# The last 256 tokens' output: copied and stored in two halves, the first while TensorE works on the second

## The reference

```python
# B, H, S, D = 4, 8, 576, 64; tokens = B*S = 2304; d_model = 512; d_ff = 2048
x = attention_with_memory(q, k, v, M_prev, z_prev, beta)    # (2304, 512)
h = x @ w_in1;  g = where(h >= 1, h, where(h <= -1, 0, (h + 1)**2 / 4));  x = g @ w_out1
h = x @ w_in2;  g = maximum(0.01 * h, h);                                 out = g @ w_out2
```

## Time and profile before

| | |
|---|---|
| median of 3 runs | 1002.1 us (1001.63 to 1003.18) |
| the profiled execution | 1002.58 us |
| its span, first to last instruction | 1000.8 us |
| PE busy | 992.4 us (99% of the span) |
| DVE, ACT, POOL busy | 446.2, 512.6, 425.4 us |
| last product ends, copies start, stores are issued | 995.72, 995.75, 996.47 us |

### The profile page before, as it was taken

The page is one execution under the profiler, slowest core; times in us unless marked ns, Lnnn a source line. Parts: engine busy times, 40 slices in busy tenths (PEclk is TensorE's granted clock), DMA queues, the critical chain, the costliest instruction groups (busy, mean ns, idle before and its releaser), DMA issues.

```text
span 1000.8 us, 16729 instructions
## 1 busy us (share of the span) xinstructions
PE 992.4 (99%) x6236; PEld 872.1 (87%) x6236; DVE 446.2 (45%) x1117; ACT 512.6 (51%) x1120; POOL 425.4 (43%) x375
## 2 busy tenths in 40 slices
PE   9999999999999999999999999999999999999997
PEld 6889999989999999999999998888888888888897
DVE  6788756666657656666422274112111111211111
ACT  6787776867677676767534374222222222322121
POOL 3478656564554546455422286222222222222221
PEclk9999999999999999999999999999999999999999
DMA  7762322332313324132110453002000200200010
GB/s 223 221 185 78 92 61 64 81 79 70 91 50 83 81 59 103 50 83 61 39 45 22 119 197 105 22 1 60 5 22 0 64 22 1 64 1 1 1 43 22
DMA packets 98290, 66.77 MB, mean 67 GB/s; under 512 B 74272, under 2 KB 87840, under 8 KB 98208
## 3 DMA queue, kind: packets, MB, share of 16 engines
q1 hardware_dynamic: 96896, 61.23, 22.4%
q10 hardware_dynamic: 1312, 4.46, 1.3%
HBM read 54.53 MB, written 11.07 MB: 66 GB/s over the span
## 4 chain that ended last, share of the span: by engine, by line
PE 90%; ACT 2%; POOL 2%; issue 2%; DVE 2%; DMA 1%; ACTq 0%; DVEq 0%; POOLq 0%
PE Hp L715 13%; PE Hp L716 13%; PE Hp L717 13%; PE Yp L739 7%; PE Yp L740 7%; PE Yp L745 7%; PE At L739 6%; PE At L740 6%; PE At L745 6%; PE At L636 4%; PE At L664 4%; PE At L555 3%; PE At L606 1%; ACT prob L773 1%; POOL Gl L1387 1%
## 5 line engine op out<-in xcount | busy, mean ns | idle before, releaser
L1387 POOL TENSOR_TENSOR Gl<-Gl_raw,Gh 128x512 fp32r<-128x512 f32 x144 | 192.3, 1336 | 435.9 <-ACT Gh L980 435.7
L715 PE MATMUL Hp<-Xh,WAh 128*128 128x256 f32 (+1 forms) x704 | 214.6, 305 | 0.0
L716 PE MATMUL Hp<-Xl,WAh 128*128 128x256 f32 (+1 forms) x704 | 212.7, 302 | 0.0
L717 PE MATMUL Hp<-Xh,WAl 128*128 128x256 f32 (+1 forms) x704 | 212.6, 302 | 0.0
L1221 DVE TENSOR_TENSOR Gl_raw<-Hp,Gl_raw 128x512 f32<-128x512 f32 x72 | 49.8, 692 | 297.5 <-ACT Gl_raw L972 297.5
L972 ACT ACTIVATE Gl_raw<-Hp 128x512 f32<-128x512 f32 x72 | 43.1, 598 | 230.4 <-PE Hp L717 230.4
L715 PEld LDWEIGHTS Hp<-Xh,WAh 128*128 128x128 f32 x704 | 134.0, 190 | 8.3 <-issue 0.4
L716 PEld LDWEIGHTS Hp<-Xl,WAh 128*128 128x128 f32 x704 | 134.1, 191 | 7.7
L980 ACT ACTIVATE Gh<-Gl_raw 128x512 fp32r<-128x512 f32 x144 | 90.9, 631 | 94.1 <-DVE Gl_raw L1221 52.3
L717 PEld LDWEIGHTS Hp<-Xh,WAl 128*128 128x128 f32 x704 | 134.0, 190 | 5.0
L739 PE MATMUL Yp<-WBh,Gh 128*128 128x512 f32 x320 | 132.5, 414 | 0.0
(11 more groups left out here) (159 smaller groups left out, 1936.3 us busy)
## 6 DMA issues: line engine op xcount, KB each, us to landing
raw<-long SPq DMA_DIRECT2D x16, 480.0 KB, 4.0
WAl_raw<-w_in SPq DMA_DIRECT2D x12, 512.0 KB, 4.9
WBl_raw<-w_out SPq DMA_DIRECT2D x12, 512.0 KB, 3.8
Vs_raw<-v_long SPq DMA_DIRECT2D x16, 320.0 KB, 3.6
yT_scratch<-xraw SPq DMA_DIRECT2D x36, 128.0 KB, 2.5
prob<-yT_scratch SPq DMA_DIRECT2D x9, 512.0 KB, 4.2
out<-prob SPq DMA_DIRECT2D x34, 128.0 KB, 2.2
bc<-rn_scratch SPq DMA_DIRECT2D x32, 128.0 KB, 3.3
```

Of the source, the lines that this page charges most:

```text
L715: pe.matmul(h, WAh[:, f, j, :], xh, start=(j == 0), stop=False)
L716: pe.matmul(h, WAh[:, f, j, :], xl, start=False, stop=False)
L717: last = pe.matmul(h, WAl[:, f, j, :], xh, start=False, stop=(j == DT - 1))
L1387: gp.tensor_tensor(Gl[:, U % 2, :], act[:, U % 2, :], Gh[:, U % 2, :].bitcast(F32), ALU.subtract).then_inc(g_lo, 1)
```

## The change

For the last unit of all (`ends`), `output` takes the products in another order: first the two pairs from `Gh` of t = 0 (tick 0), then, after the wait for `g_lo`, the two products from `Gl` of t = 0, the last of which raises the new semaphore `first_done`; then the two pairs and the two low products of t = 1. DVE waits for `first_done` and copies `Yp[:, 0, :]` (semaphore `first_out`); ACT copies `Yp[:, 1, :]` at the end (`y_out`). `store_last(eng, t, e)` now is one store: the 64 partitions 64e to 64e + 63 of one half `y2[:, t, :]`, to a view of `out` with the two batches outermost and the 32 positions inside. SP issues e = 0 and ACT e = 1, each once for t = 0 and once for t = 1.

```diff
-        def store_last(eng, t):
-
-            for e in range(2):
-                r, row = 2 * BLOCK * e + BLOCK * t, 2 * C + BLOCK * e
-                eng.dma_start(out.rearrange("(b q) d -> q b d", b=B)[row:row + BLOCK, 2 * t:2 * t + 2, :],
-                              y2[r:r + BLOCK, 0:2, :]).then_inc(out_stored, 16)
+        def store_last(eng, t, e):
+
+            row = 2 * C + BLOCK * e
+            eng.dma_start(out.rearrange("(b t q) d -> t b q d", b=2, t=2)[t, :, row:row + BLOCK, :],
+                          y2[2 * BLOCK * e:2 * BLOCK * e + 2 * BLOCK, t, :]).then_inc(out_stored, 16)
...
             def store_group(i):
+                if i == LAST:
+                    sp.wait_ge(first_out, 1)
+                    store_last(sp, 0, 0)
+                    sp.wait_ge(y_out, 2 * LAST + 1)
+                    store_last(sp, 1, 0)
+                    return
...
-                else:
-                    store_last(sp, 0)
...
                 pe.wait_ge(g_lo if tick else g_hi, U + 1)
-                for t, a in high[3:] if tick else high[:3]:
+                ends = U == 2 * CHUNKS * UNITS - 1
+
+                early = high[:2] if ends else high[:3]
+                if tick and ends:
+                    for t, a in early:
+                        last = pe.matmul(Yp[:, t, :], Gl[:, U % 2, C * a + P * t:C * a + P * t + P], WBh[:, 2 * u + a, :], start=False, stop=(a == 1))
+                    last.then_inc(first_done, 1)
+                for t, a in high[len(early):] if tick else early:
...
-                for t, a in high if tick else []:
+                for t, a in high[2 if ends else 0:] if tick else []:
...
             def group_out(i):            # ACT
+                if i == LAST:
+                    sc.wait_ge(out_stored, stores(i - 1))
+                    sc.wait_ge(first_out, 1)
+                    store_last(sc, 0, 1)
                 sc.wait_ge(y_done, FIRST_UNIT[i + 1])
...
-                    sc.wait_ge(out_stored, stores(i - 1))
-                    sc.activation(y2[:, 0, :], Yp[:, 0, :], ACT.Copy).then_inc(y_out, 1)
-                    sc.wait_ge(y_out, 2 * i + 2)
-                    store_last(sc, 1)
+                    sc.activation(y2[:, 1, :], Yp[:, 1, :], ACT.Copy).then_inc(y_out, 1)
+                    sc.wait_ge(y_out, 2 * i + 1)
+                    store_last(sc, 1, 1)
...
             def group_out(i):            # DVE
+                if i == LAST:
+                    ve.wait_ge(first_done, 1)
+                    ve.wait_ge(out_stored, stores(i - 1))
+                    ve.tensor_copy(y2[:, 0, :], Yp[:, 0, :]).then_inc(first_out, 1)
+                    return
...
-                else:
-                    ve.wait_ge(out_stored, stores(i - 1))
-                    ve.tensor_copy(y2[:, 1, :], Yp[:, 1, :]).then_inc(y_out, 1)
```

More of the change, by code:

```diff
@@ L256, in build @@
         chunk_in, x_hi, x_lo = sem("chunk_in"), sem("x_hi"), sem("x_lo")
-        h_done, relu_done, act_done, g_done, g_hi, g_lo, y_done = (sem(x) for x in ("h_done", "relu_done", "act_done", "g_done", "g_hi", "g_lo", "y_done"))
-        y_out, y_stored, out_stored = sem("y_out"), sem("y_stored"), sem("out_stored")
+        h_done, relu_done, act_done, g_done, g_hi, g_lo, y_done, first_done = (sem(x) for x in ("h_done", "relu_done", "act_done", "g_done", "g_hi", "g_lo", "y_done", "first_done"))
+        y_out, first_out, y_stored, out_stored = sem("y_out"), sem("first_out"), sem("y_stored"), sem("out_stored")
         block = ctx.enter_context(nc.Block())
@@ L506, in store_group @@
                                      yout[BLOCK * b:BLOCK * b + BLOCK, :, :, :].rearrange("p j t c -> p j (t c)")).then_inc(y_stored, 16)
-                elif is_double(i):
+                else:
                     for h in range(2):
```

## The result

The changed kernel takes 1011.02 us (median of 4 runs, 1010.6 to 1013.11), the kernel before 1002.13 (4 runs, 1001.63 to 1003.18): ratio 1.0091, 95% interval 1.0079 to 1.0103. It is slower by about 9 us, where 8.0 were forecast (1010.1 us, range 1007.5 to 1017.5). The profiled execution took 1010.6 us, its span is 1008.8.

What follows compares the result with a forecast made beforehand. TensorE bounds the span (busy 992.4 of 1000.8 us), a transfer its tail. Traffic from 996.50, 11.4 us on two engines, plus 0.89 ends the span at 1008.8, 8.0 later; on the 1002.1 median 1010.1 us, range 1007.5 to 1017.5.

Steps and rivals of the forecast that it cites:

- The form decides, 2 engines: Final stores: with 2 batches outermost at the destination, both queues' stores share the same 2 DMA engines; chance 0.62 at 1010.1 us.
- TensorE's wait: Last unit: the wait for `g_lo` before the fifth product holds TensorE 0.18 us, hidden behind the first stores' traffic.
- DVE's copy: Last unit, first half: copy from 994.58, 0.69 us, to 995.27, before the last product ends.
- Start of traffic: First final stores: data moves 1.21 us after the issue at 995.29, so from 996.50.
- The rate: Final stores: each of two engines moves 262,144 bytes at 23 GB/s, 11.4 us of traffic.
- the end after the traffic: End of the kernel: 0.89 us from the end of traffic to the end of the span, as before.
- ACT's issue: ACT's early store: its issue takes 0.38 to 0.45 us, or 0.58, leaving ACT free at 995.87 at the latest.
- The cover that I called thin: ACT free at 995.87 at the latest, before its second-half copy at 995.94; otherwise that copy is late by the difference.
- The slow rate: Rival on the final stores: two engines at 14.1 to 16.5 GB/s each, 1014.6 to 1017.3 us; chance 0.20.
- Four engines: Rival on the final stores: SP's on two engines, ACT's on two others, 5.7 us of traffic, 1004.4 us; chance 0.07.
- Sixteen: Rival on the final stores: all 16 engines serve them and the change gains 1.0 to 1.7 us; chance 0.11.

Runs made afterwards that it cites:

- outermost64: Changed kernel, but each final store's destination is 64 rows in one piece (64 outermost), same sources and moments; 1001.03 us, ratio 0.9984 to the kernel before.
- outermost4: Changed kernel, but each final store's destination is 16 positions of all four batches, batches outermost (4); 1007.09 us, ratio 1.004 to the kernel before.
- outermost8: Changed kernel, but each final store's destination is 64 rows of one batch dealt out with 8 outermost; 1003.04 us, ratio 1.0009 to the kernel before.
- rows32: Changed kernel, but each final store is cut into two of 32 partitions, one batch each (32 outermost); 1001.37 us, ratio 0.9989 to the kernel before.
- sp_alone: Changed kernel, but SP issues all four final stores and ACT none; 1010.78 us, ratio 1.0088 to the kernel before.
- form_alone: Kernel before, with its order of products and copies, but the four final stores in the changed kernel's form; 1012.6 us, ratio 1.0096 to the kernel before.
- late_pair: Changed kernel without the two early stores (first half of the last chunk's output not stored); 1007.51 us, ratio 1.0054 to the kernel before.
- no_gap: Changed kernel plus four extra two-engine stores from an idle tile to scratch, meant to be still running when the real ones join; 1014.52 us (one run).

## Why the prediction was right, step by step

- *The form decides, 2 engines.* Shown. The row that carried it was L415's share of 0.28 in a window of 0.38 us: same kind of view, wide source, four entries outermost. outermost64 and outermost4 show that it was read rightly. The rule of the Trainium skill ("DMA: Bandwidth & Descriptors", section "Why a DMA increments its semaphore by 16 and not by 1") agrees with every run here: 2, 4, 8 and 16 engines by the share, the same ones for both queues. Which engines they are no view shows, and the source has 32 or 64 outermost in every run, so a small number there is untried.
- *TensorE's wait*: 0.18 forecast, and read wrongly. The 0.21 idle is the weight loader's (PEld), which until then works one product ahead. Its load comes where forecast, 1.34 us after GpSimd's start (1.35). But the fifth product itself starts 992.72 - 991.33 = 1.39 us after that start, and before it was 993.74 - 992.35 = 1.39: no delay at all. The last product ends 3.42 after it in place of 3.37, so the order costs TensorE 0.05 us and not 0.18, and DVE's copy comes 0.13 earlier than forecast. Hidden either way.
- *Start of traffic*: 1.21 us after the issue forecast, from L415's form; after, 994.15 to about 995.4, 1.2. Right.
- *The rate, the term that was mis-sized.* I took one engine at 23 GB/s, 11.4 us. It was 12.65 (995.4 to 1008.06): 6 us at 34 or so on average, then 51 GB/s, 25.5 each, and one engine alone at the end. The lone straggler of the earlier trace rows was the end of a burst, and so a row for the second part only. That is +1.25; the start (-0.1) and the end after the traffic (0.74 in place of 0.89) take 0.2 back, and the tail is 9.0 longer, not 8.0. That the span is 1008.8 as forecast is an accident: this execution was 1.0 us ahead when GpSimd began its last subtraction.
- *ACT's issue*: 0.58 at most was forecast, it took 1.39, and ACT's copy started 0.90 after TensorE's end. The cover that I called thin was gone, but a longer one lay behind it, the queued traffic. ACT's first issue takes 1.40 and 1.45 us in outermost4 and outermost8, 0.54 in outermost64 and 0.36 to 0.45 for a store in rows32, so it goes with less than 16 engines. But only the first: ACT's second, beside SP's second and on the same engines, takes 0.53 to 0.62, and sp_alone's four issues from SP 0.51 to 0.76. No run has ACT issue alone, so SP's part in it is not shown.
- *Rivals.* The slow rate was half right: form_alone has 32 GB/s for 6 us and sp_alone 30 for 5, 15 to 16 an engine, inside that rival's 14.1 to 16.5, and the changed kernel about 17 for 6 us. It does not last: later stores from the same partitions run at 25.5 each, so the rival's price, 15.9 to 18.6 us of traffic, was too high. The page "SBUF — State Buffer" of the Trainium skill, section "Door 1: The DMA port swizzle", would by the prediction's reading cap two engines on partitions 32 apart at one port's 27.2 GB/s; the trace has 51 for 6 us and does not agree, if the engines read the two blocks side by side, which no row shows. Four engines: excluded by the share, and by sp_alone. Sixteen: right in its gain (1.2) once the form allows it.

## What to carry to other kernels

Before a store is reshaped, look at which dimension of the destination is outermost. With 32 and 64 there nothing was lost here; 2, 4 and 8 lost 9.0, 4.7 and 0.8 us of tail against the kernel before (16 itself, numbers between, and a small outermost dimension at the source were not tried). A view that puts two batches in front takes 14 of 16 engines away and shows no other sign in the code. The profile shows it in two places: a DMA share far below 1, here 0.13 to 0.45, in a window that holds only that transfer, and an issue line without a landing. And a gain of 1.2 us from overlap can be there in full and be buried under 10.3 from a side effect of the same edit: change order and form one at a time.

## What was not expected of the hardware

- Stores to two engines start slowly: 30 to 38 GB/s for 3 to 6 us, against a steady 50 to 51.
- ACT's first issue onto fewer than 16 engines, beside SP's, holds ACT for 1.2 to 1.45 us (late_pair 1.22, changed kernel 1.39), against 0.54 on 16; its second does not (0.53).
- ACT's first store onto two engines starts to move data 4.9 us after its issue in the changed kernel (994.21 to about 999.1) and in no_gap (995.20 to about 1000.1), SP's 1.2 us after. On 16 engines, in outermost64, it was 1.75 us.
